# Attention and two dense layers on one core: weight and x loads placed differently around the hand-over, with a third raw-weight and output slot

## The chip, the cores and the metric

One core of one Trainium2 chip runs the whole program. The metric is the device time of one execution in microseconds (us), lower is better. The kernel before takes 1049.78 us in the median of three runs (1048.77 to 1049.87).

## The reference

Three stages on float32 data. Attention with 4 batches, 8 heads, 576 positions and head size 64, masked by blocks of 64:

```python
scores = scale * np.matmul(q, k.transpose(0, 1, 3, 2))
scores = np.where(block_i >= block_j, scores, -1e9)
attn = exp(scores - max); attn = attn / (sum(attn) + 1e-09)
x = np.matmul(attn, v)          # laid out as 2304 tokens x 512
h = x @ w_in;  g = h * np.clip(h + 3.0, 0.0, 6.0) / 6.0;  x = g @ w_out      # 512 -> 2048 -> 512
h = x @ w2_in; g = h * np.tanh(log1p(exp(h)));            out = g @ w2_out   # 512 -> 2048 -> 512
```

## The kernel before

Every operand of a matmul is split in two parts (hi, the value rounded to TensorE's fp32r, and lo, the rest), and each product is a sum of two or three matmuls. GpSimd (POOL) splits k, q and v, ScalarE (ACT) does the exponentials and the hi parts, VectorE (DVE) does the row maxima, the lo parts and the copies out of PSUM, and SyncE (SP) issues nearly all transfers, in one hand-written order.

**Attention.** `attention_step(n)` exists once per engine and runs for n from -3 to 31 (32 heads, NHEAD = 32, HEADS = 8 per batch). In step n TensorE (PE) ends the scores of head n+1, transposes the last probabilities of head n, starts the scores of head n+2, and does the products with v for head n in two halves (`attend(n, 0)`, one tile of 128 columns, L426, and `attend(n, 1)`). DVE's `copy_o` (L770) brings the two halves into `ostage[n % 2]`, and SP's `store_o` (L275) writes them to `attn_t` in DRAM. `copy_o(n, 0)` waits until the store of head n-2 has landed (L775), since there are two output slots. In the first half of a step DVE runs, in this order, the lo part of tile 3 of head n, `copy_o(n, 0)`, and the lo part of tile 2 (L786 to L789), for which `attend(n, 1)` waits.

After the last head of a batch PE turns the row sums (`turn_sums`, L446, after `attend(n, 1)`), DVE inverts them at the end of its step (`invert_sums`, L778), and `attend` of the next head waits for that (L435), since they share a PSUM bank. SP's `store_rinv` (L282) writes the inverses to `r_d`.

On POOL a step is: k hi, q hi (`split_k_hi`, `split_q_hi` for head n+3), v hi for head n+1, q lo, v lo, k lo (L960 to L973). SP's `load_qk(n + 6)` waits for that k lo (L264), and `load_v(n + 3)` comes right behind it.

**Dense blocks.** 2304 tokens are six blocks of 384, twice (layer 0, layer 1). A block has 16 weight tiles f. In iteration f PE does `h_matmuls(f + 3)` (12 matmuls, L484) and `y_matmuls(f)` (12 matmuls, L497). Between them ACT applies the nonlinearity (L701), DVE multiplies (L860), and both split g (L674, L827); `y_matmuls(f)` waits for that lo part. In block 0 of layer 0 iteration f also splits weight tile f+4: `split_w_hi` on ACT (L629), `split_w_lo` on DVE (L811). ACT's order in an iteration is the nonlinearity of f, g hi of f-1, the weight split. DVE's is g of f, g lo of f-1, the weight split.

**Raw weights** (512 KB each, w_in and w_out side by side) pass through two slots `wraw[f % 2]`: `load_w` (L296) waits until tile m-2 is split. Tiles 0 to 3 are split in steps -1, 0, 2 and 3 (`EARLY_W`, L235). SP loads tiles 0 and 1 ahead of the steps, 2 to 5 in steps 0, 1, 6 and 7 (L333), the rest after the attention.

**x of the dense part.** `load_x` (L302) brings four column groups c of a block, each with one transfer of the two half results from `attn_t` and two broadcasts from `r_d`. Block 0 is loaded in SP's step 12, all four groups (12 transfers) in front of that step's `store_o` (L335 to L338). POOL adds and scales them (`add_x`, L979) in steps 28 (c = 0, 1) and 29 (c = 2, 3), ACT takes the hi parts in steps 29 (0, 1) and 30 (2, 3), POOL the lo parts in steps 29 (0) and 30 (1 to 3) (L232 to L234). Block 1 is loaded after the last head, all four groups, and only then weight tile 6 and on:

```python
            attention_stored(2)
            for c in range(DC):
                load_x(0, (1, None), c)
            for f in range(6, FT):
                load_w(0, f)
```

**Hand-over.** In step 31 PE runs `h_matmuls` of tiles 0 and 1 between the pieces of attention, then `turn_sums`, tile 2, and the dense loop.

Of the kernel before, what the change touches and what calls it, by code (L numbers as in the profile page):

```python
# [6 lines left out]
ACT = mybir.ActivationFunctionType  # L7
# [37 lines left out]
QK = 3  # L45
PT_ORDER = (0, 1, 3, 2)
# [3 lines left out]
def build(nc, qk, v_main, v_tail, w, w2, out):  # L50
    ctx = ExitStack()
    with ctx:
# [14 lines left out]
        wraw = [sb(f"wraw{s}", [P, 2 * D], F32) for s in range(2)]  # L67
# [10 lines left out]
        ostage = [t[:, 0:SEQ] for t in late]  # L78
# [75 lines left out]
        o_stored = [sem(f"o_stored{s}") for s in range(2)]  # L154

        w_loaded = [sem(f"w_loaded{s}") for s in range(2)]
# [99 lines left out]
        def _(sp):  # L256
# [18 lines left out]
            def store_o(n):  # L275
                sp.wait_ge(o_copied, AV * (n + 1))
                head, t0 = n % HEADS, n // HEADS * SEQ
                for half in range(2):
                    sp.dma_start(attn_t[half, head * DH:(head + 1) * DH, t0:t0 + SEQ],
                                 ostage[n % 2][half * DH:(half + 1) * DH, :]).then_inc(o_stored[n % 2], 16)  # L280
# [9 lines left out]
            def attention_stored(batches):  # L290

                for s in range(2):
                    sp.wait_ge(o_stored[s], 32 * (HEADS // 2) * batches)
                sp.wait_ge(rinv_stored, 16 * NT * batches)

            def load_w(layer, f):  # L296
                m = layer * FT + f
                if m >= 2:
                    sp.wait_ge(w_lo, m - 1)
                sp.dma_start(wraw[f % 2][:, :], (w, w2)[layer][f, :, :]).then_inc(w_loaded[f % 2], 16)  # L300
# [78 lines left out]
        def _(pe):  # L379
# [71 lines left out]
            def attention_step(n):  # L451
                last_step = n == NHEAD - 1
# [8 lines left out]
                if last_step:  # L461
                    h_matmuls((0, None), 0)
                if in_use(n + 1):
                    scores(n + 1, 4)
                if in_use(n):
                    attend(n, 0)
                if last_step:
                    h_matmuls((0, None), 1)
                if in_use(n + 2):
                    scores(n + 2, 0)  # L470
                if in_use(n + 1):
                    prob_transposes(n + 1, 0)
                    prob_transposes(n + 1, 1)
                if in_use(n + 2):
                    scores(n + 2, 1)
                if in_use(n):
                    attend(n, 1)
                    if n % HEADS == HEADS - 1:
                        turn_sums(n // HEADS)
# [55 lines left out]
            for f in range(2, LEAD):  # L535
                h_matmuls((0, None), f)
# [26 lines left out]
        def _(act):  # L563
# [37 lines left out]
            def attention_step(n):  # L601
# [24 lines left out]
                if n in EARLY_W:  # L626
                    split_w_hi(0, EARLY_W[n])

            def split_w_hi(layer, f):  # L629
                m = layer * FT + f  # L630
                act.wait_ge(w_loaded[f % 2], 16 * (m // 2 + 1))
# [4 lines left out]
                elif f == FT // 2:  # L636
                    act.wait_ge(av_done, AV * NHEAD)
                    for s in range(2):
                        act.wait_ge(o_stored[s], 32 * NHEAD // 2)
                nc.scalar.activation(w_part(whi, f, 0, 2 * D), wraw[f % 2][:, :], ACT.Copy).then_inc(w_hi, 1)  # L640
# [86 lines left out]

            dense_block(0, (0, None), (0, (1, None)))
# [15 lines left out]
        def _(dve):  # L744
# [25 lines left out]
            def copy_o(n, half):  # L770
# [3 lines left out]
                if half == 0 and n >= 2:  # L774
                    dve.wait_ge(o_stored[s], 32 * (n // 2))  # L775
                nc.vector.tensor_copy(ostage[s][:, c0:c0 + w], bank(AV_BANK[half], w)).then_inc(o_copied, 1)
# [8 lines left out]
            def attention_step(n):  # L785
                if in_use(n):  # L786
                    split_probs_lo(n, 3)
                    copy_o(n, 0)
# [9 lines left out]
                if in_use(n):  # L798
                    copy_o(n, 1)
                if in_use(n + 2):  # L800
# [7 lines left out]
                if in_use(n) and n % HEADS == HEADS - 1:  # L808
                    invert_sums(n // HEADS)

            def split_w_lo(layer, f):  # L811
                m = layer * FT + f
                dve.wait_ge(w_hi, m + 1)
                nc.vector.tensor_tensor(w_part(wlo, f, 0, 2 * D), wraw[f % 2][:, :],
# [83 lines left out]

            dense_block(0, (0, None))
# [11 lines left out]
        def _(pool):  # L911
# [48 lines left out]
            def attention_step(n):  # L960
                if n + 3 == 0:
                    split_k_lo(0)
                elif in_use(n + 3):
                    split_k_hi(n + 3)
                    split_q_hi(n + 3)
                if in_use(n + 1):
                    split_v_hi(n + 1)
                if in_use(n + 3) and n + 3 > 0:
                    split_q_lo(n + 3)
# [78 lines left out]
```

## Time and profile before

| | us |
|---|---|
| median of three runs | 1049.78 |
| the profiled execution, its own time | 1053.14 |
| its span (first to last instruction) | 1051.0 |
| PE busy | 1006.2 (96%) |
| DVE busy | 660.5 (63%) |
| ACT busy | 531.2 (51%) |
| POOL busy | 280.6 (27%) |
| mean granted TensorE clock | 0.982 |

Attention lasts to about 238 us, layer 0 to about 650, layer 1 to the end. Matmuls overlap, and their ends are modelled, so a PE that is shown busy all the time in attention need not be at its peak. The granted clock is a share of 2.4 GHz; at the level 0.5 it is 1.2 GHz.

### The profile page before, as it was taken

How to read it: one execution, taken by the hardware profiler on the slowest of the kernel's cores; microseconds unless marked ns; L12 is line 12 of the kernel's file. 1: busy time of each engine (PE TensorE's matmuls, PEld its weight loads, DVE VectorE, ACT ScalarE, POOL GpSimd, SP SyncE). 2: the span in 40 equal slices, each digit the busy share in tenths (PEclk: the TensorE clock that was granted, in tenths of full speed). 3: DMA queues.
4: the chain of work that ended last, by engine and by line, in shares of the span. 5: the costliest groups of instructions: out<-in, count | busy, mean ns of one | idle time of the engine just before them, and what ended most of it. 6: DMA issues, size and time to landing. Idle time of an engine off the chain costs nothing.

```text
span 1051.0 us, 16900 instructions
## 1 busy us (share of the span) xinstructions
PE 1006.2 (96%) x5700; PEld 939.6 (89%) x5700; DVE 660.5 (63%) x1280; ACT 531.2 (51%) x1161; POOL 280.6 (27%) x296
## 2 busy tenths in 40 slices
PE   5899699986999999999999999999999999999998
PEld 4778588876999999999999999899999999999996
DVE  5888488854623222222222457988888889888886
ACT  5888489863523232232222446555555555555553
POOL 5888489870602213022030110100101001000000
PEclk8999799988999999999999999999999999999999
DMA  7676857626512112021010233101001010000000
GB/s 191 184 187 172 222 123 182 156 52 181 178 34 75 46 36 82 2 75 45 30 63 0 98 121 134 50 8 38 24 1 45 15 37 22 0 30 0 31 1 31
DMA packets 42261, 78.89 MB, mean 75 GB/s; under 512 B 8032, under 2 KB 27616, under 8 KB 42208
## 3 DMA queue, kind: packets, MB, share of 16 engines
q1 hardware_dynamic: 36080, 68.48, 23.6%
q10 hardware_dynamic: 6128, 9.73, 2.6%
q8 instruction: 29, 0.48, 0.2%
q14 instruction: 24, 0.20, 0.1%
HBM read 59.24 MB, written 18.95 MB: 74 GB/s over the span
## 4 chain that ended last, share of the span: by engine, by line
PE 86%; DVE 3%; DMA 3%; SPq 3%; POOL 3%; issue 1%; ACT 1%; POOLq 0%; DVEq 0%; ACTq 0%
PE psum L517 37%; PE psum L494 12%; PE psum L492 12%; PE psum L493 12%; PE psum L442 4%; PE psum L421 3%; PE psum L397 3%; PE psum L402 3%; DMA attn_t<-late 2%; SPq L312 1%; POOL gsplit L933 1%; POOL klo L943 1%; DMA wraw<-in_w 1%; DMA qkin<-in_qk 0%; SPq L309 0%
## 5 line engine op out<-in xcount | busy, mean ns | idle before, releaser
L989 POOL TENSOR_TENSOR xlo<-xraw,xhi 128x384 f32 (+1 forms) x48 | 58.5, 1220 | 607.1 <-ACT xhi L649 607.1
L860 DVE SCALAR_TENSOR_TENSOR gbuf<-ebuf,psum 128x384 f32<-128x384 f32 x96 | 53.0, 552 | 222.2 <-ACT ebuf L701 222.2
L701 ACT ACTIVATE ebuf<-psum,three 128x384 f32<-128x384 f32 x96 | 55.8, 581 | 243.5 <-PE psum L494 243.5
L674 ACT ACTIVATE gsplit<-gbuf 128x384 fp32r<-128x384 f32 x192 | 100.2, 522 | 57.5 <-DVE gbuf L881 53.4
L492 PE MATMUL psum<-xhi,whi_early 128*128 (+1 forms) x384 | 129.2, 336 | 0.0
L494 PE MATMUL psum<-xhi,wlo_late 128*128 (+1 forms) x384 | 129.0, 336 | 0.0
L494 PE MATMUL psum<-xhi,wlo_early 128*128 (+1 forms) x384 | 129.0, 336 | 0.0
L492 PE MATMUL psum<-xhi,whi_late 128*128 (+1 forms) x384 | 129.0, 336 | 0.0
L493 PE MATMUL psum<-xlo,whi_late 128*128 (+1 forms) x384 | 128.7, 335 | 0.0
L493 PE MATMUL psum<-xlo,whi_early 128*128 (+1 forms) x384 | 128.7, 335 | 0.0
L827 DVE SCALAR_TENSOR_TENSOR gsplit<-gbuf,gsplit 128x384 fp32r<-128x384 f32 x192 | 122.2, 637 | 4.2 <-ACT gsplit L674 3.5
L517 PE MATMUL psum<-gsplit,whi_early 128*128 128x384 f32 x384 | 98.8, 338 | 8.3 <-DVE gsplit L827 8.3
L708 ACT ACTIVATE late<-ebuf,two 128x384 f32<-128x384 f32 x96 | 59.2, 617 | 88.1 <-DVE ebuf L844 88.0
L591 ACT ACTIVATE prob<-psum,negmax 128x128 f32<-128x128 f32 (+4 forms) x160 | 90.2, 566 | 16.5 <-DVE negmax L762 13.8
L517 PE MATMUL psum<-whi_early,gsplit 128*128 128x512 f32 x288 | 97.7, 393 | 0.5 <-DVE gsplit L827 0.5
L517 PE MATMUL psum<-whi_late,gsplit 128*128 128x512 f32 x288 | 97.7, 394 | 0.1
L517 PE MATMUL psum<-gsplit,whi_late 128*128 128x384 f32 x384 | 97.6, 335 | 0.0
L397 PE MATMUL psum<-gsplit 128*128 128x128 f32 (+2 forms) x192 | 74.7, 393 | 14.1 <-DVE gsplit L751 8.8
L517 PEld LDWEIGHTS psum<-gsplit,whi_early 128*128 128x128 f32 x384 | 70.3, 190 | 8.7 <-DVE gsplit L827 8.6
L492 PEld LDWEIGHTS psum<-xhi,whi_late 128*128 128x128 f32 x384 | 72.2, 188 | 2.1
L492 PEld LDWEIGHTS psum<-xhi,whi_early 128*128 128x128 f32 x384 | 72.3, 188 | 2.0
L493 PEld LDWEIGHTS psum<-xlo,whi_late 128*128 128x128 f32 x384 | 72.1, 188 | 2.1
(88 smaller groups left out, 2320.6 us busy)
## 6 DMA issues: line engine op xcount, KB each, us to landing
wraw<-in_w SPq DMA_DIRECT2D x32, 512.0 KB, 3.4
qkin<-in_qk SPq DMA_DIRECT2D x43, 288.0 KB, 4.4
attn_t<-late SPq DMA_DIRECT2D x64, 144.0 KB, 3.3
xraw<-attn_t SPq DMA_DIRECT2D x24, 384.0 KB, 3.4
ystage<-in_qk SPq DMA_DIRECT2D x20, 288.0 KB, 4.4
xraw<-r_d SPq DMA_DIRECT2D x48, 96.0 KB, 3.3
x_t<-ystage ACTq DMA_DIRECT2D x24, 192.0 KB, 1.9
xraw<-x_t SPq DMA_DIRECT2D x24, 192.0 KB, 2.3
```

The lines of the kernel that those rows point to most:

```text
L397: pe.matmul(bank(pb, w), q_tile, khi[s][:, k0:k0 + w], start=True, stop=False)
L492: pe.matmul(bank(f % HB, TB), hi, x_part(xhi, blk, c), start=(c == 0), stop=False)
L493: pe.matmul(bank(f % HB, TB), hi, x_part(xlo, blk, c), start=False, stop=False)
L494: last = pe.matmul(bank(f % HB, TB), lo, x_part(xhi, blk, c), start=False, stop=(c == DC - 1))
L517: last = pe.matmul(bank(4 + c, Y_COLS[layer]), stat, mov, start=(f == 0 and m == 0), stop=(f == FT - 1 and m == 2), skip_group_check=True)
L591: nc.scalar.activation(dst, src, ACT.Exp, bias=negmax[s][:, i:i + 1], accum_out=rowsum[n // HEADS % 2][:, col:col + 1]).then_inc(exp_done, 1)
L674: nc.scalar.activation(ghi[f % GS][:, :], gbuf[f % 2][:, :], ACT.Copy, scale=(1.0 / 6.0 if layer == 0 else 1.0)).then_inc(g_hi, 1)
L701: nc.scalar.activation(ebuf[f % 2][:, :], bank(f % HB, TB), ACT.Relu, bias=three[:, 0:1]).then_inc(act_ready, 1)
L708: nc.scalar.activation(rbuf[f % 2][:, :], ebuf[f % 2][:, :], ACT.Ln, bias=two[:, 0:1]).then_inc(ln_ready, 1)
L827: nc.vector.scalar_tensor_tensor(out=glo[f % GS][:, :], in0=gbuf[f % 2][:, :], scalar=(1.0 / 6.0 if layer == 0 else 1.0), in1=ghi[f % GS][ ...
L860: nc.vector.scalar_tensor_tensor(out=gbuf[f % 2][:, :], in0=e, scalar=6.0, in1=h, op0=ALU.min, op1=ALU.mult).then_inc(g_ready, 1)
L989: nc.gpsimd.tensor_tensor(x_part(xlo, blk, c), xraw[c][:, 0, :], x_part(xhi, blk, c).bitcast(F32), ALU.subtract).then_inc(x_lo, 1)
```

## The change

- Output slots `ostage` and their semaphores go from 2 to 3 (OS), raw weight slots from 2 to 3 (WS). `copy_o(n, 0)` waits for the store of head n-3, `load_w` of tile m for the split of tile m-3.
- Tiles 0 and 1 are split in steps 3 and 6, tile 2 in step 31, tile 3 right after the steps. SP loads tiles 0 to 4 in steps 0, 1, 2, 5 and 8, after `store_o`.
- SP loads x of block 0 one group at a time, in steps 11, 13, 15 and 17, after `store_o`. After the steps it issues tiles 5 and 6 first, then for each group of block 1's x one more weight tile.
- All four x hi parts and all four x lo parts of block 0 are in step 30.
- PE turns the sums before `scores(n + 2, 1)` and `attend(n, 1)`, except in step 31; DVE inverts them right after `copy_o(n, 1)`. In step 31 only tile 0's h is computed between the pieces, before `attend(31, 0)`; tiles 1 and 2 follow the step. DVE's step 31 has its own order, and `invert_sums` of the last batch comes after the lo part of tile 3.
- POOL takes the hi part of v first in its step, and q lo directly after q hi.

```diff
-        EARLY_HI = {NHEAD - 3: (0, 1), NHEAD - 2: (2, 3)}
-        EARLY_LO = {NHEAD - 3: (0,), NHEAD - 2: (1, 2, 3)}
-        EARLY_W = {-1: 0, 0: 1, 2: 2, 3: 3}
+        EARLY_HI = {NHEAD - 2: (0, 1, 2, 3)}
+        EARLY_LO = {NHEAD - 2: (0, 1, 2, 3)}
+        EARLY_W = {3: 0, 6: 1}
+        LAST = NHEAD - 1
...
-                if m >= 2:
-                    sp.wait_ge(w_lo, m - 1)
+                if m >= WS:
+                    sp.wait_ge(w_lo, m + 1 - WS)
...
             load_v(0)
-            load_w(0, 0)
             load_qk(2)
             load_v(1)
-            load_w(0, 1)
...
-                if n in (0, 1, 6, 7):
-                    load_w(0, 2 + (0, 1, 6, 7).index(n))
-                if n == HEADS + 4:
-                    attention_stored(1)
-                    for c in range(DC):
-                        load_x(0, (0, None), c)
                 if in_use(n):
                     store_o(n)
                     if n % HEADS == HEADS - 1:
                         store_rinv(n // HEADS)
+                if n in (0, 1, 2, 5, 8):
+                    load_w(0, (0, 1, 2, 5, 8).index(n))
+                if n in (11, 13, 15, 17):
+                    if n == 11:
+                        attention_stored(1)
+                    load_x(0, (0, None), (n - 11) // 2)
+            load_w(0, 5)
+            load_w(0, 6)
             attention_stored(2)
             for c in range(DC):
                 load_x(0, (1, None), c)
-            for f in range(6, FT):
+                load_w(0, 7 + c)
+            for f in range(7 + DC, FT):
                 load_w(0, f)
...
-                if last_step:
-                    h_matmuls((0, None), 0)
-                if in_use(n + 1):
-                    scores(n + 1, 4)
+                if in_use(n + 1):
+                    scores(n + 1, 4)
+                if n == LAST:
+                    h_matmuls((0, None), 0)
                 if in_use(n):
                     attend(n, 0)
-                if last_step:
-                    h_matmuls((0, None), 1)
...
+                if n != LAST and in_use(n) and n % HEADS == HEADS - 1:
+                    turn_sums(n // HEADS)
...
-            for f in range(2, LEAD):
+            for f in range(1, LEAD):
                 h_matmuls((0, None), f)
...
+                if n == LAST:
+                    split_w_hi(0, 2)
...
+            split_w_hi(0, 3)
             dense_block(0, (0, None), (0, (1, None)))
...
-                if half == 0 and n >= 2:
-                    dve.wait_ge(o_stored[s], 32 * (n // 2))
+                if half == 0 and n >= OS:
+                    dve.wait_ge(o_stored[n % OS], 32 * (n // OS))
...
+                if n == LAST:
+                    split_probs_lo(n, 2)
+                    copy_o(n, 0)
+                    split_w_lo(0, 2)
+                    copy_o(n, 1)
+                    return
...
                 if in_use(n):
                     copy_o(n, 1)
+                    if n % HEADS == HEADS - 1:
+                        invert_sums(n // HEADS)
...
+            split_w_lo(0, 3)
+            invert_sums(BATCH - 1)
             dense_block(0, (0, None))
...
-                elif in_use(n + 3):
+                if in_use(n + 1):
+                    split_v_hi(n + 1)
+                if in_use(n + 3) and n + 3 > 0:
                     split_k_hi(n + 3)
                     split_q_hi(n + 3)
-                if in_use(n + 1):
-                    split_v_hi(n + 1)
-                if in_use(n + 3) and n + 3 > 0:
                     split_q_lo(n + 3)
```

## Rows read from the trace of the kernel before

**Rows 1.** Chain that ended last, whole run: start us, us, what.

```profile
248.54 6.76 DMA wraw<-in_w
258.62 3.80 PE psum L517 x12
...
643.06 2.08 PE psum L517 x12
```

**Rows 2.** Longest waits, 0 to 262 us: in total, times, longest us.

```profile
DVE late L776 <- DMA attn_t<-late: 15.0, 9, 8.4
...
PE psum L517 <- DVE gsplit L827: 8.3, 1, 8.3
...
PE psum L442 <- DVE rinv L782: 2.3, 3, 0.8
```

**Rows 3.** DVE timeline, `copy_o(n, 0)` of heads 0, 1, 11 to 15.

```profile
22.43 0.28 DVE L776 COPY late<-psum 128x128 f32<-128x128 f32 x1
...
29.45 0.28 DVE L776 COPY late<-psum 128x128 f32<-128x128 f32 x1
...
95.23 0.29 DVE L776 COPY late<-psum 128x128 f32<-128x128 f32 x1
...
101.01 0.29 DVE L776 COPY late<-psum 128x128 f32<-128x128 f32 x1
...
108.21 0.29 DVE L776 COPY late<-psum 128x128 f32<-128x128 f32 x1 [1.38 <-DMA attn_t<-late]
...
122.18 0.29 DVE L776 COPY late<-psum 128x128 f32<-128x128 f32 x1 [8.37 <-DMA attn_t<-late]
...
131.53 0.29 DVE L776 COPY late<-psum 128x128 f32<-128x128 f32 x1 [1.04 <-PE psum L442]
```

**Rows 4.** Chain that ended last, 100 to 140 us: start us, us, what.

```profile
105.19 1.40 POOL klo L943
...
108.46 0.47 SPq L273
...
116.88 5.21 DMA attn_t<-late
```

**Rows 5.** Timelines of ACT, PE and DVE at the start, 13 to 30 us.

```profile
14.31 1.04 ACT L640 ACTIVATE whi_early<-wraw 128x1024 fp32r<-128x1024 f32 x1
...
13.29 0.30 PE L397 MATMUL psum<-gsplit 128*128 128x128 f32 x1 [0.27 <-issue]
...
16.89 0.69 PE L397 MATMUL psum<-gsplit 128*128 128x384 f32 x1 [2.07 <-ACT prob L591]
...
22.18 0.42 PE L397 MATMUL psum<-gsplit 128*128 128x128 f32 x1
...
27.92 1.22 DVE L814 TENSOR_TENSOR wlo_early<-wraw,whi_early 128x1024 fp32r<-128x1024 f32 x1
```

**Rows 6.** Stretch of 5 us: busy us (x) by engine, then PEclk, DMA share, GB/s.

```profile
75.00:80.00 5.00, 4.43 (x24) 4.06 (x24) 2.84 (x7) 3.00 (x11) 4.71 (x6) 0.75 0.93 264
```

**Rows 7.** Timelines of PE and POOL in steps 28 to 31.

```profile
222.06 0.69 PE L397 MATMUL psum<-gsplit 128*128 128x384 f32 x1 [3.06 <-ACT prob L591]
...
231.48 0.42 PE L492 MATMUL psum<-xhi,whi_early 128*128 128x384 f32 x1
...
224.37 1.00 POOL L985 TENSOR_TENSOR xraw<-xraw 128x384 f32<-128x384 f32 x1
...
227.63 2.94 POOL L989 TENSOR_TENSOR xlo<-xraw,xhi 128x384 fp32r<-128x384 f32 x3
```

**Rows 8.** Timelines of DVE and SP at the hand-over.

```profile
238.22 0.94 DVE L782 RECIPROCAL rinv<-psum 40x128 f32<-40x128 f32 x1
...
239.49 1.86 SPq L287 DMA_DIRECT2D r_d<-rinv  x5
```

**Rows 9.** DMA issues, whole run: count, KB each, median us to landing.

```profile
wraw<-in_w SPq DMA_DIRECT2D x32, 512.0 KB, 3.4
...
vin<-in_v_tail SPq DMA_DIRECT2D x32, 16.0 KB, 3.8
```

More of the change, by code:

```diff
@@ L45 @@
 QK = 3
+OS = 3
+WS = 3
 PT_ORDER = (0, 1, 3, 2)
@@ L66, in build @@
         wlo = [sb("wlo_early", [P, FT // 2, 2 * D], F32R)]
-        wraw = [sb(f"wraw{s}", [P, 2 * D], F32) for s in range(2)]
+        wraw = [sb(f"wraw{s}", [P, 2 * D], F32) for s in range(WS)]
         xraw = [sb(f"xraw{c}", [P, 3, TB], F32) for c in range(DC)]
@@ L77, in build @@
         tbuf, qbuf = (late[1][:, s * TB:(s + 1) * TB] for s in range(2))
-        ostage = [t[:, 0:SEQ] for t in late]
+        ostage = [t[:, 0:SEQ] for t in late] + [sb("ostage", [P, SEQ], F32)]
         wbuf = sb("wbuf", [P, TB], F32)
@@ L153, in build @@
         o_copied = sem("o_copied")
-        o_stored = [sem(f"o_stored{s}") for s in range(2)]
-        w_loaded = [sem(f"w_loaded{s}") for s in range(2)]
+        o_stored = [sem(f"o_stored{s}") for s in range(OS)]
+        w_loaded = [sem(f"w_loaded{s}") for s in range(WS)]
         w_hi = sem("w_hi")
@@ L232, in build, with stored @@
         EARLY_ADD = {NHEAD - 4: (0, 1), NHEAD - 3: (2, 3)}
-        EARLY_HI = {NHEAD - 3: (0, 1), NHEAD - 2: (2, 3)}
-        EARLY_LO = {NHEAD - 3: (0,), NHEAD - 2: (1, 2, 3)}
-        EARLY_W = {-1: 0, 0: 1, 2: 2, 3: 3}
+        EARLY_HI = {NHEAD - 2: (0, 1, 2, 3)}
+        EARLY_LO = {NHEAD - 2: (0, 1, 2, 3)}
+        EARLY_W = {3: 0, 6: 1}
+        LAST = NHEAD - 1
+        def stored(s, heads):
+            return 32 * -((s - heads) // OS)
         def pt_source(u):
@@ L279, in store_o @@
                     sp.dma_start(attn_t[half, head * DH:(head + 1) * DH, t0:t0 + SEQ],
-                                 ostage[n % 2][half * DH:(half + 1) * DH, :]).then_inc(o_stored[n % 2], 16)
+                                 ostage[n % OS][half * DH:(half + 1) * DH, :]).then_inc(o_stored[n % OS], 16)
             def store_rinv(b):
@@ L290, in attention_stored @@
             def attention_stored(batches):
-                for s in range(2):
-                    sp.wait_ge(o_stored[s], 32 * (HEADS // 2) * batches)
+                for s in range(OS):
+                    sp.wait_ge(o_stored[s], stored(s, HEADS * batches))
                 sp.wait_ge(rinv_stored, 16 * NT * batches)
@@ L297, in load_w @@
                 m = layer * FT + f
-                if m >= 2:
-                    sp.wait_ge(w_lo, m - 1)
-                sp.dma_start(wraw[f % 2][:, :], (w, w2)[layer][f, :, :]).then_inc(w_loaded[f % 2], 16)
+                if m >= WS:
+                    sp.wait_ge(w_lo, m + 1 - WS)
+                sp.dma_start(wraw[m % WS][:, :], (w, w2)[layer][f, :, :]).then_inc(w_loaded[m % WS], 16)
             def load_x(layer, blk, c):
@@ L637, in split_w_hi @@
                     act.wait_ge(av_done, AV * NHEAD)
-                    for s in range(2):
-                        act.wait_ge(o_stored[s], 32 * NHEAD // 2)
-                nc.scalar.activation(w_part(whi, f, 0, 2 * D), wraw[f % 2][:, :], ACT.Copy).then_inc(w_hi, 1)
+                    for s in range(OS):
+                        act.wait_ge(o_stored[s], stored(s, NHEAD))
+                nc.scalar.activation(w_part(whi, f, 0, 2 * D), wraw[m % WS][:, :], ACT.Copy).then_inc(w_hi, 1)
             def split_x_hi(layer, blk, c):
@@ L773, in copy_o @@
                 dve.wait_ge(av_done, AV * n + half + 1)
-                if half == 0 and n >= 2:
-                    dve.wait_ge(o_stored[s], 32 * (n // 2))
-                nc.vector.tensor_copy(ostage[s][:, c0:c0 + w], bank(AV_BANK[half], w)).then_inc(o_copied, 1)
+                if half == 0 and n >= OS:
+                    dve.wait_ge(o_stored[n % OS], 32 * (n // OS))
+                nc.vector.tensor_copy(ostage[n % OS][:, c0:c0 + w], bank(AV_BANK[half], w)).then_inc(o_copied, 1)
             def invert_sums(b):
@@ L807, in attention_step @@
                     split_w_lo(0, EARLY_W[n])
-                if in_use(n) and n % HEADS == HEADS - 1:
-                    invert_sums(n // HEADS)
             def split_w_lo(layer, f):
@@ L968, in attention_step @@
                 if in_use(n + 3) and n + 3 > 0:
+                    split_k_hi(n + 3)
+                    split_q_hi(n + 3)
                     split_q_lo(n + 3)
```

12 lines of the change are left out of this document (5 added, 7 removed).

## The prediction

> **What bounds the kernel now.** I read the chain of waits first. From 258.62 us it is matmuls alone: twelve y matmuls take 2.08 us in every iteration down to 643 us [rows 1], and in the second layer the spacing is as even. Nothing in the change touches that stretch, except that layer 1's raw weights get a slot more, and PE does not wait for them. So the money is in the first 262 us. There I looked at the waits, at the granted clock of short stretches, and at when DVE starts the copy of each head's first half, as a beat of the attention steps.
>
> An undisturbed step lasts 101.01 - 95.23 = 5.78 us [rows 3]. The 32 copies show where more is paid. The worst place is steps 12 to 14: the intervals ahead of heads 14 and 15 are 13.97 and 9.35 us [rows 3]. The chain shows why: SP ends its v loads at 108.93, then issues twelve x transfers, and the second half of head 12's store goes out at 116.88 and takes 5.21 us to land [rows 4]; the copy of head 14 needs that slot and waits 8.37 us [rows 3]. The second large hole is the hand-over. Tile 6 is issued at 248.54, behind block 1's x, lands 6.76 us later, and PE waits 8.3 us for a g lo part that is queued behind its split on ACT and DVE; the y matmuls after it take 3.80 us for 2.08, at the low clock [rows 1, 2]. The third hole is a wait of 3.06 us in step 30 [rows 7].
>
> **The change, part by part** (gains against the profiled execution).
>
> *x of block 0 spread out.* Each of four steps gets 3 transfers after its store. The twelve took about 7.2 us (108.93 to the store), so 1.8 us each. Undisturbed, SP is idle for some 2.2 us of a step: 5.78 less six issues of some 0.6 us (two for q and k, two for v, two for the store; the v tail takes 0.47, rows 4). Cover: that idle time; in step 15 five `r_d` stores (1.86 us, rows 8) come on top and SP runs about 1.5 us late, which the third slot and the loads' lead absorb. If the cover fails, four steps lose 1.8 each, 7 us. Gain: 8.19 + 3.57 = **11.8 us**, including the half-speed clock behind the hole [rows 3].
>
> *Third output slot.* All waits of the copies for stores are 15.0 us in nine places, of which 8.4 is the one above [rows 2]. The other 6.6 us go away, as a store gets 5.78 us more. I take **6.0**; between 3 (if the next wait, PE or ACT, was only just hidden) and 6.6. The row of head 13 has such a wait, 1.38 us, with no x load in its way, and its interval is 7.20 us, 1.42 too long [rows 3]. The Trainium skill speaks against this part: "DMA: Bandwidth & Descriptors", section "Anatomy of one DMA", fits 2.0 us plus bytes at 436 GB/s to a transfer, on GpSimd's path. By it a 144 KB store lands in 2.3 us, two slots would be enough, and this term would be about 0, the sum 6 us smaller. The trace has the wait, so the rows decide.
>
> *Weight splits out of the steps.* One costs 1.04 us on ACT and 1.22 on DVE [rows 5]; both are near full in a step. The price by the beat is 7.02 - 5.78 = 1.24 us [rows 3]. The splits of steps 0 and 2 go, that of step 3 stays, step 6 gets one: net **1.2**, between 0 and 2.5. Tiles 2 and 3 move to where ACT and DVE have gaps (below).
>
> *Start.* Tile 0's split sits in front of ACT's work for PE at 14.31; PE then waits 2.07 us, falls to the low clock, and the step takes 22.18 - 13.29 = 8.89 us instead of 5.78 [rows 5]. Without it the wait is about 1.0 us, nearer to the 0.8 of the longest wait for an inverse [rows 2], which by itself cost no slow stretch at the later batch ends. The lo split (1.22 us) goes too, and 1 MB of the start's transfers. 3.1 is the ceiling, 1.0 (the ACT time alone, low clock kept) the floor; I take **2.5**.
>
> *Batch ends.* DVE's 0.94 us inverse [rows 8] stays in the step. PE's wait for it goes (2.3 us in three places, rows 2), but DVE is as late as before with everything behind it. I take 0; between 0 and 2.3. After the first batch end the clock is 0.75 for 5 us, that is 2.5 us at 1.2 GHz [rows 6]. Two of the three waits ahead of it go, so I count half of 2.5, **1.2**; 0 if it stays.
>
> *POOL's order.* v hi moves into POOL's wait for PE. It takes 0.45 us out of the way of q lo and k lo: 0 in the steps, as POOL is not what they wait for; 0.45 us in step 28 to 31. But it now waits first for v, see the second rival.
>
> *Steps 28 to 31.* ACT no longer stops in step 29 for x. PE's step 29 ended at 222.06 - 3.06 = 219.0 [rows 7]; step 30 now keeps its beat, and without scores of a next head it ends at about 224 instead of 230. But POOL's own work is unchanged: its scaling ends at 225.37 [rows 7], about 224.8 with the 0.45 us. In step 30 ACT now takes hi of c = 3 only after that, and head 31's exponentials are behind it: PE waits from 224 to about 227. After v's splits (1.3 us) POOL does four lo parts where it did three in 2.94 us [rows 7]: 224.8 + 1.3 + 3.9 = 230.0. `h_matmuls(0)` needs them all; it started at 231.48 [rows 7]. So the stall moves by one step and 1.5 us are gained. Since PE has stood still twice before 230, its h runs at the low clock at first. The rows at either level (3.80 against 2.08 us, rows 1) make the price of a restart on dense matmuls 1.7. Net **0** (-0.2, rounded), from a gain of 3 to a loss of 3.
>
> *Hand-over.* PE's order has the same work, so the end of `attend(31, 1)` comes at about A = 235.4, being 230.0 + 2.1 (tile 0) + 1.75 (attend) + 1.6. DVE then copies (0.8), splits tile 3 (1.15), and inverts: A + 2.9. SP stores the inverses, 0.3 + 1.86 + 0.2 us [rows 8], and issues tile 5 at A + 5.2. With the median landing of 3.4 [rows 9] it is there at A + 8.6; from landing to the y matmul took 258.62 - 255.30 = 3.3 us [rows 1], so y of f = 1 can start at A + 11.9. PE is ready for it after three h, one y and one h, A + 0.3 + 5 x 2.08 = A + 10.7. New wait: 1.2 us, in place of 8.3 plus 1.7 of slow clock. Tile 6 lands some 2 us later and needs 4 us less urgently; the others have a whole turn of three iterations, 12.5 us, for a landing of 3.4 to 6.8. Gain 10.0 - 1.2 = **8.8**; with a landing of 6.76 as before, the wait is 4.6 and may drop the clock (1.7): 3.7. With no wait, 10.0.
>
> **Sum**: 11.8 + 6.0 + 1.2 + 2.5 + 1.2 + 0 + 8.8 = 31.5 us. The profiled execution took 1053.1 us, so it would take 1021.6; the median of the runs is 3.4 us lower, and I take the same difference from it: 1049.8 - 31.5 = **1018** us.
>
> **Rivals.**
> 1. *The stalls move to the hand-over.* Every gain in the steps stands, but x's POOL chain and tile 5's load (behind the inverse, five small stores and the last head's stores) end last: step 31 loses 3, and the hand-over keeps 3.7 of its 8.8. Then 1018 + 3 + 5.1 = 1026. For it: tile 5 cannot be asked for before tile 2 is split in step 31, and SP meets `store_rinv` first. Against: nothing else is on the queues then.
> 2. *POOL, SP and the v load become the beat, and the kernel is slower.* v hi of step n+2 stands first on POOL, and waits for a load issued in step n after k lo. k lo ended at 106.59, the tail of v was issued at 108.46 [rows 4]: 1.87 us later. With the landing L, then about 5.65 us of POOL work (a step less its wait for PE) up to the next k lo but one, two steps cannot be shorter than 7.52 + L. At the median L = 3.8 [rows 9] that is 5.66 us a step, just under 5.78; k hi used to be first and gave v 1.3 us more. It decides at L = 4.0. At 4.8 all along, a step is 6.16: 28 x 0.38 = 11 us, 1029. Slower than before needs L above 6.3 (28 steps x 1.13 us); at 6.5 it is 28 x 1.23 = 34 us and 1052. For: near the x burst stores took 5.21 us [rows 4], and x loads still fall in four steps. Against: that was twelve transfers in a row, and steps without them are the rule.
> 3. *The steps hide nothing more.* The holes close, but another wait of the same length is right behind, so only the burst and the hand-over pay: 11.8 + 8.8, 1029. Against: undisturbed steps are seen in numbers, and have the same ACT and DVE work.
>
> **How the numbers follow.** My forecast 0.6, rival 1 0.15, rival 2 in its mild form 0.09 and in its slower form 0.03, rival 3 0.08, all undone to no change 0.02, and the rest of faster cases 0.03. The case's own bounds: upward the 3 of the third slot, 1.5 at the start, 1.2 each for splits and clock and part of 7 from SP, not all together, to 1026; downward 2.3 + 3 + 1.2 + 1.3 + 0.6 + 0.6, to 1009. The mild forms of the rivals reach to 1029, so the range is 1009 to 1031. A measurement here tells 0.2% (2 us) from nothing; faster 0.95, same 0.02, slower 0.03.
>
> **What would show it.** In the profile after: no wait of a copy for a store; copies 5.8 us apart from head 9 to 30 but for batch ends; granted clock 1.00 from about 25 to 220 us; a PE wait for ACT in step 30 or 31, and h of tile 0 not before POOL's last x lo; one PE wait of 1 to 2 us in dense iteration 1 with tile 5's landing behind it; the y matmuls of layer 1 as before, only 31 us earlier. I am wrong if steps 11 to 17 are longer than 6.2 us (SP or DMA), if POOL waits for v in most steps (rival 2), or if PE waits over 4 us at the hand-over (rival 1).

## The result and the profile after

The changed kernel takes 1022.23 us (median of four runs, 1021.7 to 1023.85) against 1049.82 (1048.77 to 1050.3): a ratio of 0.9741, with a 95% interval of 0.9724 to 0.9758, or 27.6 us less. The forecast was 1018 in a range of 1009 to 1031. One run of the kernel before that took 1119.76 us, at a mean clock of 0.841, counts in none of the ratios and intervals of this document.

| | before | after |
|---|---|---|
| median of the runs, us | 1049.8 | 1022.2 |
| the profiled execution, its own time | 1053.1 | 1022.1 |
| its span | 1051.0 | 1020.3 |
| PE busy | 1006.2 (96%) | 995.0 (98%) |
| mean granted TensorE clock | 0.982 | 0.997 |

DVE's timeline of `copy_o(n, 0)` of heads 0, 1 and 11 to 16 in the changed kernel, beside [rows 3]:

```profile
19.03 0.29 DVE L787 COPY late<-psum 128x128 f32<-128x128 f32 x1
...
25.03 0.29 DVE L787 COPY late<-psum 128x128 f32<-128x128 f32 x1
...
86.37 0.29 DVE L787 COPY ostage<-psum 128x128 f32<-128x128 f32 x1
...
92.13 0.29 DVE L787 COPY late<-psum 128x128 f32<-128x128 f32 x1
...
97.89 0.29 DVE L787 COPY late<-psum 128x128 f32<-128x128 f32 x1
...
103.65 0.29 DVE L787 COPY ostage<-psum 128x128 f32<-128x128 f32 x1
...
110.05 0.29 DVE L787 COPY late<-psum 128x128 f32<-128x128 f32 x1 [0.68 <-PE psum L451]
...
117.41 0.27 DVE L787 COPY late<-psum 128x128 f32<-128x128 f32 x1
```

I call the time from the copy of one head to that of the next the interval of the later head. It is 5.76 us through heads 12 to 14 now, where 9.6 us were lost (1.4 at head 13, 8.2 at head 14), and no copy waits for a store. The start is 3.4 us earlier (22.43 to 19.03). But heads 15 and 16 have intervals of 6.40 and 7.36 us, and two more like them (heads 19 and 20, 6.37 and 6.88) follow. The wait table (0 to 262 us) has a line that the table of the kernel before does not have. POOL waits for v:

```profile
POOL vs L971 <- DMA vin<-in_v_tail: 7.7, 9, 2.3
```

PE's waits of over 0.4 us from 200 us on, in its timeline:

```profile
205.73 1.84 PE L430 MATMUL psum<-ident,prob 64*128 64x64 f32 x9 [2.55 <-ACT prob L599]
208.85 0.69 PE L500 MATMUL psum<-xhi,whi_early 128*128 128x384 f32 x1 [1.28 <-POOL xlo L1008]
...
225.23 0.62 PE L525 MATMUL psum<-gsplit,whi_early 128*128 128x384 f32 x2 [0.45 <-DVE gsplit L845]
```

and POOL's four lo parts of x in its own timeline:

```profile
204.93 3.86 POOL L1008 TENSOR_TENSOR xlo<-xraw,xhi 128x384 fp32r<-128x384 f32 x4
```

The wait of 3.06 us in step 30 [rows 7] has moved to the head of step 31 (2.55), a second one stands in front of tile 0's h, and of the 8.3 us at the hand-over 0.45 is left. The stretch table shows what follows the two waits: the first matmuls of the dense part run at 1.2 GHz (columns as in [rows 6]).

```profile
205.00:210.00 5.00, 2.99 (x13) 2.48 (x14) 2.34 (x5) 3.51 (x6) 3.79 (x4) 0.50 0.25 59
210.00:215.00 5.00, 5.00 (x28) 4.93 (x27) 2.19 (x4) 1.62 (x3) 0.00 (x0) 0.83 0.01 3
```

From tile 0's h on PE has the same work in both traces. To the end it takes 1051.0 - 231.5 = 819.5 us before and 1020.3 - 208.9 = 811.4 after, and the 8.1 between them are the hand-over's, with the slow first matmuls taken off.

### The profile page after: what moved, and what is told of

It is laid out like the page before. It is cut to its first block, busy times and chain, and to the rows that moved or that the text cites. A ratio compares the mean times of both kernels' runs of the same rounds, so it can differ in the third digit from the quotient of the medians.

```text
span 1020.3 us, 16901 instructions
## 1 busy us (share of the span) xinstructions
PE 995.0 (98%) x5700; PEld 931.1 (91%) x5700; DVE 662.3 (65%) x1280; ACT 530.9 (52%) x1161; POOL 279.7 (27%) x296
## 4 chain that ended last, share of the span: by engine, by line
PE 90%; DVE 4%; POOL 2%; issue 2%; ACT 1%; DMA 1%; SPq 0%; DVEq 0%; POOLq 0%
PE psum L525 38%; PE psum L500 13%; PE psum L502 13%; PE psum L501 13%; PE psum L451 4%; PE psum L430 4%; PE psum L406 3%; PE psum L411 3%; DMA qkin<-in_qk 0%; PE psum L409 0%; ACT prob L599 0%; POOL xraw L1002 0%; POOL xlo L1008 0%; DVE gsplit L845 0%; DVE wlo_early L832 0%
## 5 line engine op out<-in xcount | busy, mean ns | idle before, releaser
L406 PE MATMUL psum<-gsplit 128*128 128x128 f32 (+2 forms) x192 | 71.5, 377 | 12.2 <-DVE gsplit L762 8.7
L501 PEld LDWEIGHTS psum<-xlo,whi_early 128*128 128x128 f32 x384 | 72.5, 189 | 1.9
```

What stands on the lines that cost most here:

```text
L406: pe.matmul(bank(pb, w), q_tile, khi[s][:, k0:k0 + w], start=True, stop=False)
L501: pe.matmul(bank(f % HB, TB), hi, x_part(xlo, blk, c), start=False, stop=False)
```

## The experiments

Each states the median of its own runs (in brackets the lowest and highest) and the ratio to the kernel before, which ran beside it on the same chip (medians 1049.1 to 1049.8), with its 95% interval. The changed kernel did not run beside them, so that a difference to its 1022.2 us (ratio 0.9724 to 0.9758) counts as clear only where the two intervals, or all the runs, lie apart. By the intervals that is so for experiments 3, 4, 8 and 11 (8 by a hair), by all the runs for 2 and 10, and not for 1, 7 and 9. Experiments 5, 6 and 12 start from the kernel before and compare with it.

**1. POOL's old order.** In the changed kernel:

```diff
+                if in_use(n + 3) and n + 3 > 0:
+                    split_k_hi(n + 3)
+                    split_q_hi(n + 3)
                 if in_use(n + 1):
                     split_v_hi(n + 1)
                 if in_use(n + 3) and n + 3 > 0:
-                    split_k_hi(n + 3)
-                    split_q_hi(n + 3)
                     split_q_lo(n + 3)
```

> The changed kernel (1022.2 us) with POOL's old order in a step: k hi, q hi, v hi, q lo. In the changed kernel POOL waits 7.7 us in nine places for v, twice over 2 us, and the copies of heads 15, 16, 19 and 20 come 6.40, 7.36, 6.37 and 6.88 us after the one before, 3.4 us too long in all (with 0.5 for the batch end taken off). Theory (v first makes POOL wait for v in two of the four x steps): the v waits vanish, those four intervals go to 5.8 (6.3 at the batch end), the time is 1018.8 us. Rival (those steps are long because all transfers are late, q and k too): POOL waits for something else and the time stays within 1 us of 1022.2. Second rival (the new order is worth its 0.45 us in every step): slower, up to 1030.

Measured: 1022.95 us (1021.8 to 1027.4), ratio 0.9754 (0.9727 to 0.9781), no difference from the changed kernel. Yet the waits went as the theory said:

```profile
POOL vs L971 <- DMA vin<-in_v_tail: 0.8, 1, 0.8
```

and the copies of heads 15, 16 and 19 came after 5.90, 6.31 and 5.89 us (head 20 still after 6.63). These four intervals give 2.3 us, and by the trace as much is paid elsewhere: six other intervals (heads 3, 11, 13, 22, 27 and 29) are 5.87 to 5.91 instead of 5.76, 0.8 us in all, the start is 0.5 us later, and step 31 is 1 us longer (13.21 for 12.22). So the new order cost 2.3 us in the x steps and gave it back in other places, and the sum is 0; that those other places come from the order, and not from the spread between executions, is not shown.

**2. v loads first in SP's step.** This removes the cause and keeps the new order.

```diff
+                if 2 <= n + 3 < NHEAD:
+                    load_v(n + 3)
                 if QK <= n + 6 < NHEAD:
                     load_qk(n + 6)
-                if 2 <= n + 3 < NHEAD:
-                    load_v(n + 3)
```

> The changed kernel (1022.2 us, v waits of POOL 7.7 us in nine places) with one swap in SP's step: the v loads of head n+3 go out in front of the q and k loads of head n+6, not behind them. q and k are asked for three steps ahead and can be later. Theory (v is late because it is issued behind 576 KB of q and k and, in the x steps, behind x too): v lands 2 to 3 us after its issue and is issued 1.2 us earlier, the waits vanish, the copies of heads 15, 19 and 20 come 5.8 us after the one before and that of 16 6.3: 3.4 us less, 1018.8. Rival (what POOL waits for is the bandwidth of all loads): the waits move to q and k, no gain.

Measured: 1020.07 us (1018.8 to 1020.2), ratio 0.9721 (0.9705 to 0.9736), 2.2 us less. No wait for v is left in the trace (v's second load lands in 2.3 us in the median, for 3.7 in the changed kernel). From head 10 to head 30 all intervals are 5.74 to 5.77 us, but for the two batch ends and the head behind each:

```profile
109.24 0.29 DVE L787 COPY late<-psum 128x128 f32<-128x128 f32 x1
115.44 0.27 DVE L787 COPY late<-psum 128x128 f32<-128x128 f32 x1
121.34 0.29 DVE L787 COPY ostage<-psum 128x128 f32<-128x128 f32 x1
```

(head 15 after 5.76, the batch end after 6.20, then 5.90.) Tile 0's h starts 3.8 us earlier than in the changed kernel (205.08), but behind a wait of 2.01 instead of 1.28 us; the clock then reads 0.50 from 205 to 210 us and 0.90 to 215, and the hand-over's wait is 0.94. So 1.9 of the 3.8 are given back there. The cause of the long x steps is shown: v was issued behind q and k, in steps in which x loads were under way.

**3. Two output slots** (`OS = 2`, the rest as changed).

> The changed kernel with two output slots instead of three, all else kept. By the prediction's term the third slot is worth 6.0 us: 1028.2, with waits of copies for stores of some 6 us again. Rival (most of those waits stood only behind the bursts of loads in front of the stores, and the stores now come first): under 2 us, 1022 to 1024. Rival of the page (a store lands in 2.3 us): 0.

Measured: 1030.13 us (1026.6 to 1034.0), ratio 0.9815 (0.9787 to 0.9843), 7.9 us more. The wait table of that trace:

```profile
DVE late L787 <- DMA attn_t<-late: 6.9, 7, 2.5
```

with heads 11, 14 and 18 after 6.79, 7.28 and 8.22 us. This profile is of the fastest of the six runs, 4.5 us above the changed kernel's, so that the third slot is worth 4.5 us by the profiled runs and 7.9 by the medians, which fits the 6.0 that I had taken; the other value, 0, is ruled out for this kernel. The Trainium skill ("DMA: Bandwidth & Descriptors", section "Anatomy of one DMA") fits 2.0 us plus bytes at 436 GB/s, on GpSimd's path; the estimate from it is 2.3 us for a store of 144 KB, which would leave no wait with two slots. The stores are on SP's path, and the trace disagrees: they landed in 3.3 us in the median before, and the copies wait 6.9 us in seven places above.

**4. The burst with three slots.** All twelve x transfers in step 12, in front of the store, in the changed kernel.

> The changed kernel with block 0's x loaded as before, all twelve transfers in step 12 in front of the store, with three output slots. If the spreading carries the 11.8 us of the burst, the time is 1030 to 1034. If the third slot alone would have caught most of it: store 12 lands at about 122 in the old count and the copy of head 15 is due at 120, so a wait of some 2 us instead of 8.4, plus POOL's wait for the late v of head 16, 3 us, minus the 3.4 us of v waits that the spread loads cost: 1022 to 1026, with the clock staying up.

Measured: 1028.9 us (1028.0 to 1031.8), ratio 0.9806 (0.9774 to 0.9839), 6.7 us more. One copy waits 1.9 us for a store instead of 8.4, but POOL waits 5.8 us for one v, and the intervals are 8.05, 8.14 and 9.68 us (heads 15 to 17).

```profile
115.35 0.45 POOL L971 CAST vs<-vin 128x320 fp32r<-128x320 f32 x1 [5.82 <-DMA vin<-in_v_tail]
```

So the slot alone takes over less than half of the 11.8 us of the burst, and both theories were too pure.

**5. x spread, in the kernel before.**

```diff
-                if n == HEADS + 4:
-                    attention_stored(1)
-                    for c in range(DC):
-                        load_x(0, (0, None), c)
...
+                if n in (11, 13, 15, 17):
+                    if n == 11:
+                        attention_stored(1)
+                    load_x(0, (0, None), (n - 11) // 2)
```

> The kernel before with one part of the change alone: x of block 0 one group at a time in steps 11, 13, 15 and 17, after the store (two output slots, old order of POOL, old hand-over). By the prediction's term 11.8 us less: 1038. With two slots a store behind loaded queues may still be waited for, some 2 us in two places: 1040 to 1042. Rival (the burst only shows a delay that comes later anyway): above 1044.

Measured: 1044.22 us (1042.5 to 1045.3), ratio 0.9934 (0.9911 to 0.9956): 5.5 us, not 11.8. The 8.4 us wait is gone, but with two slots the copies wait for stores in 11 places, 10.7 us in all, the longest 2.4; and behind the longest the clock drops again:

```profile
110.00:115.00 5.00, 2.98 (x22) 2.65 (x20) 2.57 (x7) 2.46 (x7) 3.89 (x5) 0.95 1.00 263
115.00:120.00 5.00, 5.00 (x22) 3.86 (x22) 2.61 (x6) 2.56 (x10) 1.50 (x2) 0.50 0.82 245
```

Spreading and slot are not separate: to save the whole 11.8 us takes both.

**6. Tile 6 first, in the kernel before.**

```diff
+            load_w(0, 6)
             attention_stored(2)
             for c in range(DC):
                 load_x(0, (1, None), c)
-            for f in range(6, FT):
+                load_w(0, 7 + c)
+            for f in range(7 + DC, FT):
                 load_w(0, f)
```

> The kernel before with only SP's order after the attention changed: weight tile 6 first, then for each group of block 1's x one more tile (two raw slots as before). Theory (PE's 8.3 us at the hand-over are tile 6's late issue alone, and 1.7 us more are the low clock behind it): tile 6 is issued at 241.5, lands at 245 to 246, no PE wait or under 1 us, 9 to 10 us less: 1040. Rival (two slots are too few, the next tiles then wait for the split of the one two before): a wait of 2 to 5 us in iterations 2 to 4, 1043 to 1046.

Measured: 1039.45 us (1038.5 to 1043.9), ratio 0.9891 (0.9869 to 0.9912): 10.3 us from four changed lines. The profile is of the slowest of its four runs (1043.89 us; the others took 1038.5 to 1039.6), with 2.3 us of store waits at head 8 that have nothing to do with the edit. The chain of that trace runs through the place without a gap, y matmuls every 4.16 us at full clock:

```profile
242.85 2.09 PE psum L519 x12
...
247.02 2.08 PE psum L519 x12
...
251.18 2.08 PE psum L519 x12
```

From tile 0's h to the end it takes 1041.8 - 232.4 = 809.4 us, 10.1 less than in the kernel before and 2.0 less than in the changed one. Two raw slots were enough for it: the 8.3 us wait and the 1.7 of low clock came from the order of SP's queue alone. No run takes the third raw slot by itself out of the changed kernel.

**7. The splits back at the start** (`EARLY_W = {-1: 0, 0: 1}`, the two loads ahead of the steps, the rest as changed).

> The changed kernel with tiles 0 and 1 split in steps -1 and 0 as before (and loaded as before), not in 3 and 6. Theory (the split in step -1 keeps PE at the durations of 1.2 GHz up to 22 us): the copy of head 0 comes at 22 instead of 19 us, that of head 1 7.0 to 7.5 after it instead of 6.0, and the intervals of heads 4 and 7 go from 7.21 to 5.8: 3.1 + 1.3 - 2.9 = 1.5 us more, 1023.7. Rival (the start is late or early by chance, as one variant without that split showed 22.2): the copy of head 0 at 19 or 22 as before, and 1.6 us less.

Measured: 1025.48 us (1023.1 to 1030.4), ratio 0.9778 (0.9744 to 0.9812), 3.3 us more, which the spread of its four runs does not set clearly apart from the changed kernel. Head 0's copy is at 22.30 again, head 1's 7.34 after it, and heads 4 and 7 at 5.76. PE's timeline has the long wait again that stood in [rows 5]:

```profile
16.76 0.69 PE L408 MATMUL psum<-gsplit 128*128 128x384 f32 x1 [2.18 <-ACT prob L601]
```

It starts its 384 columns with 0.69 us, the duration at 1.2 GHz; without the split that line reads 0.45 us behind a wait of 1.05. The trade by the intervals is 3.3 + 1.3 - 2.9 = 1.7 us. Heads 19 and 20 (6.70 and 8.45 us for 6.37 and 6.88) add 1.9 us in that trace, with a clock of 0.94 and 0.71 from 135 to 145 us; they stand at v waits of the x steps, not at a split.

**8. Batch ends as before**, in the changed kernel (the sums turned after `attend(n, 1)`, inverted at the end of DVE's step).

> The changed kernel with the batch ends as before: PE turns the sums after the second half of the attention product, DVE inverts them at the end of its step. My term was 0. The intervals at heads 8, 16 and 24 were 1.82, 1.40 and 1.03 us too long before (the first with 1.09 of a wait for a store in it) and 0.58, about 0.5 and 0.45 in the changed kernel. Theory (the new place hides half of the inverse): 0.3 + 0.9 + 0.6 = 1.5 to 2 us more, three PE waits of 0.77 us for the inverse again. Rival (DVE's 0.94 us cost the same anywhere): within 0.5 us.

Measured: 1024.87 us (1024.1 to 1026.6), ratio 0.9776 (0.9760 to 0.9792), 2.6 us more. The three waits are back,

```profile
PE psum L451 <- DVE rinv L791: 2.3, 3, 0.8
```

and heads 8, 16 and 24 are 6.97, 8.00 and 6.86 us behind the one before, for 6.34, 7.36 and 6.21. The heads behind them are 5.76 us apart for 5.89, so that the batch ends cost 1.5 us by the intervals and 2.6 by the medians. My term 0 was wrong by that.

**9. The scaling of x spread over steps** (`EARLY_ADD = {19: (0,), 22: (1,), 25: (2,), 28: (3,)}`).

> The changed kernel with POOL's scaling of block 0's x taken out of steps 28 and 29: one column group (2.0 us) in each of steps 19, 22, 25 and 28. Theory (POOL's chain of 8 us of scaling, v and 3.9 us of lo parts sets the start of tile 0's h, and PE stands still 2.55 + 1.28 us and then runs at 1.2 GHz for it): the chain starts 6 us earlier, both waits shrink to under 1 us, the slow stretch goes with them; gain 5 to 7 us in steps 30 and 31, less up to 0.9 us in each of three steps where POOL is late by 2.0 against a slack of 1.1: 1016 to 1020. Rival (ACT's four hi parts, 2 us, and the exponentials of the last head set it): a gain of under 2 us, and the waits turn to ACT.

Measured: 1023.44 us (1021.3 to 1026.0), ratio 0.9739 (0.9712 to 0.9766), no difference. The last step behaves as the theory says: its interval is 7.55 us instead of 12.22, the wait for ACT is 1.06 for 2.55, PE does not wait for POOL in front of tile 0, and tile 0's h starts at full clock:

```profile
212.74 1.11 PE L430 MATMUL psum<-ident,prob 64*128 64x64 f32 x9 [1.06 <-ACT prob L599]
...
213.98 0.44 PE L500 MATMUL psum<-xhi,whi_early 128*128 128x384 f32 x1
```

But five intervals behind the scaling are longer than in the changed kernel (heads 21, 22, 25, 27 and 28: 6.18, 6.88, 6.77, 6.10 and 6.89 us), 3.9 us in all, more than the 2.7 I had allowed: POOL was busy for 46.3 of the 50 us from 140 to 190 already in the changed kernel, and is for 47.8 here, so that 2.0 us of extra work are not caught up in three steps. Head 19 (7.12 us for 6.37) is longer as well, but stands before the first scaling, at a v wait of 3.01 us. This profile is of the slowest of the five runs, and its start was late too, 22.16 us, without a split in step -1; of the nine profiles without one it is the only such.

**10. Another last step**, in the changed kernel: x hi of groups 2 and 3 in ACT's step 31, their lo parts on DVE, both halves of `attend` in front of tile 0's h. Since the lo parts now come from two engines, SP waits for all four before it loads block 1's x.

```diff
-        EARLY_HI = {NHEAD - 2: (0, 1, 2, 3)}
-        EARLY_LO = {NHEAD - 2: (0, 1, 2, 3)}
+        EARLY_HI = {NHEAD - 2: (0, 1)}
+        EARLY_LO = {NHEAD - 2: (0, 1)}
...
-                    sp.wait_ge(x_lo, lin(blk, DC, c + 1 - DC))
+                    sp.wait_ge(x_lo, DC if blk == (1, None) else lin(blk, DC, c + 1 - DC))
...
-                if n == LAST:
-                    h_matmuls((0, None), 0)
...
-            for f in range(1, LEAD):
+            for f in range(0, LEAD):
...
+                if n == LAST:
+                    split_x_hi(0, (0, None), 2)
                 if in_use(n):
                     split_probs_hi(n, 3)
+                if n == LAST:
+                    split_x_hi(0, (0, None), 3)
...
                     split_probs_lo(n, 2)
+                    for c in (2, 3):
+                        dve.wait_ge(x_hi, c + 1)
+                        nc.vector.tensor_tensor(x_part(xlo, (0, None), c), xraw[c][:, 0, :],
+                                                x_part(xhi, (0, None), c).bitcast(F32), ALU.subtract
+                                                ).then_inc(x_lo, 1)
                     copy_o(n, 0)
```

> The changed kernel with another last step: ACT takes x hi of groups 2 and 3 in step 31 behind the last exponentials, DVE (idle 3.8 us there) takes their lo parts from POOL, and PE does both halves of the last attention product before tile 0's h. Theory (the 2.55 us wait is ACT's stop for the scaling of group 3, the 1.28 us wait is POOL's four lo parts, and the low clock of tile 0's h follows from both): both waits go, PE does the 1.75 us of attention while it used to stand, h of tile 0 starts at 207 us of the trace instead of 208.9 and at 2.4 GHz with attention behind it already: 4.5 to 6 us less, 1017. Rival (the gain is lost again at tile 5's load, which hangs on the last copies and the inverse): they are earlier too, so at most 1 us is lost.

Measured: 1019.49 us (1018.6 to 1020.5), ratio 0.9705 (0.9686 to 0.9724), 2.7 us less.

```profile
203.78 1.20 PE L430 MATMUL psum<-ident,prob 64*128 64x64 f32 x9 [0.24 <-ACT prob L597]
205.49 0.30 PE L451 MATMUL psum<-pthi,vs 128*128 128x128 f32 x1 [0.51 <-DVE ptlo L780]
...
206.46 0.47 PE L451 MATMUL psum<-pthi,vs 128*128 128x448 f32 x1 [0.56 <-DVE ptlo L780]
...
208.99 0.67 PE L498 MATMUL psum<-xhi,whi_early 128*128 128x384 f32 x1
```

The two waits are 0.24 and 0, and the attention is done when the h matmuls begin. But they begin at 208.99, not 207, and at 0.67 us for 384 columns: the clock came down behind the first wait and two new ones of half a microsecond for DVE's lo parts of the probabilities. It reads 0.71 from 205 to 210 us and 0.95 to 215, for 0.50 and 0.83 in the changed kernel. The combined version of experiment 11 has the same three waits and the same 0.67 us.

**11. Both, a version under both kernels.** Experiments 2 and 10 together.

> The variant with the other last step (1019.5 us, 0.9705 of the kernel before) and the v loads in front of the q and k loads. If both causes are separate they add up: 2.7 + 3.4 us under the changed kernel, 1016. If v was the cause of nothing on the path: 1019.5.

Measured: **1015.83 us** (1014.1 to 1016.0), ratio 0.9677 (0.9664 to 0.9691): 33 us under the kernel before, 6.4 under the changed one, somewhat more than the 4.9 that the two gave apart. v in front of q and k brings 3.7 us here, on top of the other last step, for the 3.4 that the intervals of the x steps had promised.

**12. The kernel before, profiled again.**

> The kernel before, unchanged, profiled once more. In the first profile it took 1053.1 us and its other runs 1049; the copy of head 0's first half came at 22.4 us, and in the profiles of the changed kernel and its variants it came at 19.0 to 19.5 four times and at 22.2 once, each time with PE's matmuls at the 1.2 GHz durations until after it in the late ones. Theory (the start has two outcomes whatever the kernel, and the profile of before happened to show the late one, so the start term of 2.5 us was taken from a profile that the median does not share): in a profile with 1048 to 1050 us the copy comes at 19 to 20.5; with 1052 to 1054 at 22 to 23. Rival (the weight split in step -1 always makes it late): 22 to 23 in any profile.

Measured: the profiled execution took 1049.67 us, its span is 1047.5, and the start is late all the same:

```profile
22.33 0.28 DVE L776 COPY late<-psum 128x128 f32<-128x128 f32 x1
...
75.96 0.29 DVE L776 COPY late<-psum 128x128 f32<-128x128 f32 x1 [0.25 <-PE psum L442]
...
82.45 0.29 DVE L776 COPY late<-psum 128x128 f32<-128x128 f32 x1 [0.80 <-DMA attn_t<-late]
```

So my theory of two outcomes of the start fell, and the rival held, though not to the letter: with a split in step -1 the copy comes at 22.43, 22.33, 22.07, 22.30 and once (experiment 5) at 21.02 us, and experiment 9 is late without one. The 3.5 us between the two profiles of one kernel are elsewhere: 2.3 of them up to the copy of head 29, 1.0 from there to tile 0's h, 0.2 behind it. Heads 8 and 9, the last two rows above, have intervals of 6.76 and 6.49 us, for 7.58 and 7.24 in the first profile. The wait table has

```profile
DVE late L776 <- DMA attn_t<-late: 13.5, 7, 8.5
...
PE psum L517 <- DVE gsplit L827: 7.4, 1, 7.4
```

for 15.0 and 8.3 [rows 2], and the stretch that read 0.75 in [rows 6] keeps its clock:

```profile
75.00:80.00 5.00, 4.49 (x33) 3.93 (x33) 4.48 (x11) 3.83 (x12) 4.71 (x6) 1.00 0.91 247
```

In step 30 PE waits as long as before for ACT, but its clock holds at first, and tile 0's h comes 14.4 us after the copy of head 29, for 15.4 in the first profile [rows 7]:

```profile
219.60 0.44 PE L397 MATMUL psum<-gsplit 128*128 128x384 f32 x1 [3.05 <-ACT prob L591]
...
228.16 0.45 PE L492 MATMUL psum<-xhi,whi_early 128*128 128x384 f32 x1 [0.23 <-POOL xlo L989]
```

The shorter wait at the hand-over gains next to nothing, since the y matmuls behind it stay slow for longer. The next twelve start 6.64 us later, for 5.88 in the first profile:

```profile
254.42 4.21 PE psum L517 x12
...
261.06 2.08 PE psum L517 x12
```

## Why the prediction was right, and where it was off

The sum of 31.5 us holds against the profiled execution that it was made for: 1053.14 - 1022.14 = 31.0. What the median shows is 27.6. **The step that failed is the last one**, "the median of the runs is 3.4 us lower, and I take the same difference from it". The profiled execution of before was not longer evenly; it was longer in places that the change touches. Experiment 12 shows them, as far as one more profile can. With its rows my terms are: slots 5.0 for 6.6 of waits (1.5 less, taken at my share), clock behind the first batch end 0 for 1.2, steps 28 to 31 1.0 less to gain, hand-over the same but for 0.1 (7.4 of wait and 2.5 of slow clock for 8.3 and 1.7): 31.5 - 3.8 = 27.7, and 1049.8 - 27.7 = 1022.1, next to the 1022.2 measured. That it is this close is partly luck, since terms below were off by up to 3.4 us and cancel.

Term by term:

- *Burst and third slot*, 11.8 and 6.0: the places were right; that the terms stand apart was wrong. Spreading alone gave 5.5 us (experiment 5); undoing only one of the two cost 6.7 and 7.9 (experiments 4 and 3). The two together are then worth some 5.5 + 7.9 = 13.4 us and not 17.8, an estimate, since one part was measured in each kernel.
- *Splits and start*, 1.2 + 2.5: the sum of 3.7 was right, by luck. The start gave 3.4 us, the splits 0.2 (intervals of heads 1, 3, 4 and 7, less head 7's wait for a store before). A split is dearer than I read from head 1's interval: 1.45 us each in the changed kernel for my 1.24. Experiment 7 moves two of the splits only, and its 1.7 us by the intervals bear out the start and this price.
- *Batch ends*, 0: mis-sized. Experiment 8: 1.5 us by the intervals, 2.6 by the runs.
- *Rival 2 in its mild form came true*, and I had left it out of the sum: POOL waited 7.7 us for v, some 3.4 of it on the path, in two of the four x steps (heads 15, 16, 19 and 20: 27.0 us for 4 x 5.76, less 0.6 for the batch end at head 16). That was one of my own signs of being wrong: heads 15 and 16 passed the 6.2 us that I had allowed in steps 11 to 17. My landing of 4.0 us as what decides held roughly: the tails of v that POOL waited for longest (2.2 and 2.3 us) landed in 5.4 and 4.9 us, most others from head 2 on in 2.0 to 4.1. Four more took 4.3 to 4.9, and no interval there is longer than a split or a batch end makes it elsewhere. Against it the batch ends (1.5) and a start better than forecast (0.9) gave back most of the 3.4.
- *Steps 28 to 31*, 0: from the copy of head 29 to tile 0's h I had 230.0 - 216.1 = 13.9 us for 15.4 before; it is 208.85 - 194.73 = 14.1. Both waits and the low clock are where they were put, and POOL's chain is the cause (experiments 9 and 10). But the 1.3 us gained before tile 0's h are lost again in its slow matmuls: the dense part is 2.0 us longer than in experiment 6, and only 0.7 of that are the hand-over's wait and the slow clock behind it.
- *Hand-over*, 8.8 with a new wait of 1.2: the wait is 0.45, tile 5 landed in 3.3 us. Experiment 6 prices the move by itself at 10.3, for the 10.0 of the estimate; less 0.7 for the new wait and its slow clock, 9.4 of the 10.1 remain.

Rivals 1 and 3 did not come about.

## What to carry to other kernels

When a queue feeds several consumers, put the load that is needed first in front: four lines in SP's order were worth 10 us at the hand-over, and v in front of q and k another 2 to 4. Work that is moved off one engine's stalled step has to be followed to the engine that feeds it; here what was gained by freeing ACT in step 29 waited one step later behind POOL's 8 us of scaling. And before a sum made on one profiled execution is taken off a median, ask whether that execution's surplus lies in the very places that are summed; a second profile of the kernel before tells. Compare there not the waits alone but the way from one fixed point to the next: a shorter wait can have a longer slow stretch behind it.

## What the runs showed of the hardware

- Waits too short to matter one by one were followed by the low clock together: waits of 0.24, 0.51 and 0.56 us, with transposes and short matmuls between them (experiment 10), stand ahead of matmuls of 0.67 us for 384 columns, which take 0.44 at full clock (experiment 9). A single wait of 0.95 to 0.97 us in the steps of the changed kernel (behind the splits and at heads 15 and 19) did not have it behind it: the clock reads 1.00 there.
- The granted clock of a stretch is not always what its matmuls ran at. Behind the split of step -1 it shows the slow stretch: 0.60 and 0.71 from 15 to 25 us in the kernel before, 0.66 and 0.66 in experiment 7, against 1.00 and 1.00 in the changed kernel. But in experiment 9 it reads 1.00 there, and the matmuls are those of 1.2 GHz up to 23.6 us. The first two rows are experiment 9's, the third is the changed kernel's:

```profile
14.98 0.56 PE L406 MATMUL psum<-gsplit 128*128 128x256 f32 x1
...
16.63 0.69 PE L406 MATMUL psum<-gsplit 128*128 128x384 f32 x1 [0.64 <-ACT prob L599]
...
14.21 0.36 PE L406 MATMUL psum<-gsplit 128*128 128x256 f32 x1
```

  Where the two differ the durations tell. They tell too that the wait of 0.64 us is not what made that start slow: the matmul ahead of it is slow already. Both traces, and that of the kernel before, begin with the durations of 1.2 GHz (0.44 us for 288 columns at 12 us, with the granted clock at 1.00). The kernel before has left them by 12.7 us and the changed kernel by 14.2, experiment 9 only by 24. Why, with PE at work for 4.97 of the 5 us from 10 to 15, stays open.
- Executions of one kernel spread over 1.4 us (experiment 2) to 7.4 (experiment 7); the kernel before took 1047.3 to 1053.6 us. In its two profiles the 3.5 us between them lie in waits at loaded transfers that differ by up to 1.1 us, and in whether, and for how long, the clock falls behind a wait.
